# Two layers' product orders written out per 16 blocks, the negative part in three reduced-precision passes in every other block, and the last product with tokens on the partitions

## The chip, the cores and the metric

The kernel runs on one core of a Trainium2 chip (trn2). The metric is the device time of one execution in microseconds (us); the time of a kernel is the median over several executions. Inside a profile the time stands as a span, from the first to the last profiled instruction, which is about 2 us shorter than the device time of the same execution.

## The reference, cut to what matters

```python
# attention: 12288 queries, 768 pooled keys, width 128      -> x (12288 x 128)
h = x @ w_in1                                   # 128 -> 2048
x = (np.maximum(h, 0.0) + alpha * np.minimum(h, 0.0)) @ w_out1      # 2048 -> 128
h = x @ w_in2                                   # 128 -> 2048
P = a[0] + a[1] * h + a[2] * h**2 + a[3] * h**3
Q = 1.0 + np.abs(b[0]) * np.abs(h) + np.abs(b[1]) * h**2
return (P / (Q + 1e-06)) @ w_out2               # 2048 -> 128, float32
```

## The kernel before

All of x is kept in SBUF as two float32r halves, `x_hi` and `x_lo` (a rounded part and the rest), with the 128 features on the partitions. The attention fills it in the first fifth of the time. Then both layers run over 24 groups of 512 tokens; a group has 16 blocks of 128 hidden features, so each layer has 384 blocks. Every engine has its own instruction queue in one fixed order, and the queues meet through semaphores.

**Layer 1, block n.** TensorE: `hidden1(n)` (three float32r passes by `split_product`, L659 to L661) into the only PSUM bank `H1`. ScalarE takes its negative part `negative(n)` (L386); every fourth block VectorE does (L615). TensorE: `out1(n)` multiplies it by `wout1` in full float32 (L818) into `ACC1`, onto a linear term (`lin_hi`, `lin_lo`) that stands in for the rest of the activation. `hidden1(n+1)` waits until the negative part of block n is out of `H1`. After 16 blocks `hidden_hi` (ScalarE) and `hidden_lo` (VectorE) write the layer's output back to `x_hi`, `x_lo`.

**Layer 2, block m**, which runs `DEPTH` = 20 blocks behind. TensorE: `hidden2(m)` into one of three PSUM banks. ScalarE: `square` (L394), `scaled_abs` (L402), `linear_part` (L408). GpSimd: `cubic_term` (L256). VectorE: `denominator` (L577), `polynomial` (L583). ScalarE: `log` (L414), `inverse_q` (L422). VectorE: `check_product` (L600), `quotient` (L591). GpSimd: `correction` (L240), `final` (L248); in every fourth block VectorE does `final` (L608) and no correction is needed. TensorE: `out2(m)` (L829), full float32, into `ACC2`, with features on the partitions. `hidden2(m)` needs the quotient of block m-3, since there are three banks; `final(m)` needs `out2(m-3)`, since `rational` has three buffers.

**The output.** After 16 blocks ScalarE copies `ACC2` to `y_t` (`copy_output`), TensorE transposes it in four parts (`turn_output`, L835), VectorE copies it out (`place_output`, L627), and SyncE stores it.

A loop over periods of four blocks (`QUAD`) writes each engine's queue.

Of the kernel before, what the change touches and what calls it, by code (L numbers as in the profile page):

```python
# [13 lines left out]
P = 128  # L14
# [7 lines left out]
QUAD = 4  # L22
DEPTH = 5 * QUAD
BY_DVE_FINAL, BY_DVE_RELU = 2, 3
# [9 lines left out]
def build(nc, q, kv, w_sr, w_in1, w_out1, alpha, w_in2, w_out2, coef_p, coef_q, out):  # L34
# [7 lines left out]
    N1 = GROUPS * BLOCKS  # L42
# [11 lines left out]
    with ctx:  # L54
# [24 lines left out]
        with ExitStack() as scope:  # L79
# [4 lines left out]
            k_hi, k_lo = att("k_hi", [P, keys], F32R), att("k_lo", [P, keys], F32R)  # L84
            v_hi, v_lo = att("v_hi", [P, CHUNKS, P], F32R), att("v_lo", [P, CHUNKS, P], F32R)
            pt_hi, pt_lo = att("pt_hi", [P, 2, GROUP], F32R), att("pt_lo", [P, 2, GROUP], F32R)
            probs, expd = att("probs", [P, 2, TILES, keys]), att("expd", [P, 2, keys])
# [4 lines left out]
        y_t, y_out = sb("y_t", [P, GROUP]), sb("y_out", [P, GROUP])  # L92
# [24 lines left out]
        for name in (  # L117
# [5 lines left out]
            "in1_t_ready", "in1_t_done", "lin_ready", "lin_hi_done", "lin_lo_done", "out1_scaled",  # L123
# [4 lines left out]
            "h1_ready", "neg_done", "neg_dve_done", "m1_done", "y1_hi_done", "y1_done",  # L128
            "h2_ready", "sq_done", "absb_done", "linp_done", "cubic_done", "poly_done", "q_done", "ln_done", "rcp_done",
            "ratio_done", "qr_done", "newton_done", "rat_done", "rat_dve_done", "m2_done", "y2_copied", "y2_t_ready", "y2_out_done",  # L130
# [10 lines left out]
        def real(m):  # L141
            return 0 <= m < N1

        def group_at(p, offset):
            g = (p - offset) * QUAD // BLOCKS
            return g if (p - offset) * QUAD % BLOCKS == 0 and 0 <= g < GROUPS else None

        def negative_ready(eng, n):

            if n >= 0 and n % QUAD == BY_DVE_RELU:  # L150
                after(eng, s["neg_dve_done"], n // QUAD + 1)
            elif n >= 0:
                after(eng, s["neg_done"], n + 1 - (n + QUAD - BY_DVE_RELU) // QUAD)

        def rational_ready(eng, m):

            if m >= 0 and m % QUAD == BY_DVE_FINAL:
                after(eng, s["rat_dve_done"], m // QUAD + 1)
            elif m >= 0:
                after(eng, s["rat_done"], m + 1 - (m + QUAD - BY_DVE_FINAL) // QUAD)  # L160

        PERIODS = N1 // QUAD + DEPTH // QUAD + 2

# [27 lines left out]
        def _(pool):  # L191
# [45 lines left out]
            def correction(m):  # L237
                if real(m):
# [35 lines left out]
        def _(act):  # L274
# [160 lines left out]
            for p in range(PERIODS):  # L435
                n, m = p * QUAD, p * QUAD - DEPTH
                if group_at(p, 10) is not None:
                    copy_output(group_at(p, 10))
# [449 lines left out]
```

## Time and profile before

| | |
|---|---|
| median of 3 runs | 1619.42 us (1613.58 to 1620.19) |
| the profiled execution | 1616.42 us, span 1614.3 us |
| busy share of the span | TensorE 96%, VectorE 88%, ScalarE 87%, GpSimd 71% |

The shares are over the whole span with the attention in it, where GpSimd does little. In the trace an operation's record is longer than the step from its start to that of the next one, because operations are pipelined; the time that an operation takes from its engine is the step. In an entry such as `banks<-x_hi,win_lo` the output stands first. A full float32 matmul is two records, a float32r one is one record.

### The profile page before, as it was taken

How to read it: one execution, taken by the hardware profiler on the slowest of the kernel's cores; microseconds unless marked ns; L12 is line 12 of the kernel's file. 1: busy time of each engine (PE TensorE's matmuls, PEld its weight loads, DVE VectorE, ACT ScalarE, POOL GpSimd, SP SyncE). 2: the span in 40 equal slices, each digit the busy share in tenths (PEclk: the TensorE clock that was granted, in tenths of full speed). 3: DMA queues.
4: the chain of work that ended last, by engine and by line, in shares of the span. 5: the costliest groups of instructions: out<-in, count | busy, mean ns of one | idle time of the engine just before them, and what ended most of it. 6: DMA issues, size and time to landing. Idle time of an engine off the chain costs nothing. (4 is left out here: it accounts for less than half of the span.)

```text
span 1614.3 us, 22125 instructions
## 1 busy us (share of the span) xinstructions
PE 1555.7 (96%) x5869; PEld 1015.0 (63%) x5869; DVE 1412.7 (88%) x2175; ACT 1398.8 (87%) x2659; POOL 1149.2 (71%) x1256
## 2 busy tenths in 40 slices
PE   6899999989999999999999999999999999999976
PEld 5799999845566565655565555656656555656532
DVE  3688888727999999999999999999999999999997
ACT  2577777628999999999999999999999999999996
POOL 0344444306888888888888888888888888888887
PEclk9999999999999999999999999999999999999998
DMA  8110100000000000000000000000000000000000
GB/s 223 53 27 21 27 21 27 1 26 1 7 1 7 8 8 7 1 7 7 7 1 8 7 8 7 1 7 7 8 1 8 7 7 8 1 7 7 7 7 7
DMA packets 12299, 24.54 MB, mean 15 GB/s; under 512 B 1536, under 2 KB 1680, under 8 KB 11920
## 3 DMA queue, kind: packets, MB, share of 16 engines
q1 hardware_dynamic: 11424, 22.55, 4.7%
q8 instruction: 46, 0.75, 0.2%
q10 hardware_dynamic: 752, 0.60, 0.1%
q14 instruction: 77, 0.63, 0.1%
HBM read 16.85 MB, written 6.29 MB: 14 GB/s over the span
## 5 line engine op out<-in xcount | busy, mean ns | idle before, releaser
L256 POOL TENSOR_TENSOR cubic<-sq,lin_p 128x512 f32<-128x512 f32 x384 | 492.4, 1283 | 225.4 <-ACT lin_p L408 178.0
L659 PE MATMUL banks<-x_hi,win_lo 128*128 128x512 f32 x768 | 508.4, 662 | 25.2 <-DVE ratio L591 15.3
L248 POOL TENSOR_TENSOR rational<-newton,ratio 128x512 f32<-128x512 f32 x288 | 368.6, 1280 | 35.8 <-PE banks L829 13.6
L818 PE MATMUL banks<-neg_part,wout 128*128 128x512 f32 x768 | 388.0, 593 | 0.3 <-ACT neg_part L386 0.3
L829 PE MATMUL banks<-rational,wout 128*128 128x512 f32 x768 | 379.2, 601 | 4.2 <-POOL rational L248 4.1
L577 DVE SCALAR_TENSOR_TENSOR banks<-sq,abs_b,banks 128x512 f32<-128x512 f32 x384 | 282.3, 752 | 59.2 <-ACT banks L402 57.2
L661 PE MATMUL banks<-x_hi,win_hi 128*128 128x512 f32 x768 | 303.7, 395 | 0.0
L660 PE MATMUL banks<-x_lo,win_hi 128*128 128x512 f32 x768 | 303.3, 395 | 0.0
L591 DVE SCALAR_TENSOR_TENSOR ratio<-banks,ab_raw,rcp 128x512 f32<-128x512 f32 x384 | 285.5, 743 | 1.3 <-ACT rcp L422 1.2
L583 DVE SCALAR_TENSOR_TENSOR banks<-banks,ab_raw,cubic 128x512 f32<-128x512 f32 x384 | 280.0, 752 | 0.0
L659 PEld LDWEIGHTS banks<-x_hi,win_lo 128*128 128x128 f32 x768 | 145.1, 189 | 205.1 <-issue 67.7
L408 ACT ACTIVATE lin_p<-banks,ab_raw 128x512 f32<-128x512 f32 x384 | 267.2, 696 | 0.0
L394 ACT ACTIVATE sq<-banks 128x512 f32<-128x512 f32 x384 | 231.1, 602 | 37.6 <-PE banks L661 37.6
L422 ACT ACTIVATE rcp<-log_q 128x512 f32<-128x512 f32 x384 | 247.9, 646 | 3.1
L414 ACT ACTIVATE log_q<-banks 128x512 f32<-128x512 f32 x384 | 231.9, 604 | 2.3 <-DVE banks L577 2.2
L402 ACT ACTIVATE banks<-banks 128x512 f32<-128x512 f32 x384 | 223.4, 600 | 0.8 <-DVE newton L600 0.6
L660 PEld LDWEIGHTS banks<-x_lo,win_hi 128*128 128x128 f32 x768 | 145.8, 190 | 123.4 <-issue 115.9
L386 ACT ACTIVATE neg_part<-banks 128x512 f32<-128x512 f32 x288 | 175.2, 608 | 39.6 <-PE banks L661 29.3
L600 DVE SCALAR_TENSOR_TENSOR newton<-banks,rcp 128x512 f32<-128x512 f32 x288 | 197.3, 686 | 10.5 <-ACT rcp L422 7.5
L829 PEld LDWEIGHTS banks<-rational,wout 128*128 128x128 f32 x768 | 146.8, 192 | 90.2 <-issue 59.9
L818 PEld LDWEIGHTS banks<-neg_part,wout 128*128 128x128 f32 x768 | 142.6, 189 | 79.3 <-issue 54.1
L240 POOL TENSOR_SCALAR newton<-newton 128x512 f32<-128x512 f32 x288 | 178.0, 618 | 0.9 <-DVE newton L600 0.9
(84 smaller groups left out, 1891.1 us busy)
## 6 DMA issues: line engine op xcount, KB each, us to landing
early<-in_kv_dram SPq DMA_DIRECT2D x24, 256.0 KB, 9.6
out_dram<-y_out SPq DMA_DIRECT2D x24, 256.0 KB, 2.0
neg_part<-in_q_dram SPq DMA_DIRECT2D x22, 256.0 KB, 2.6
early<-in_moe_w_in_dram SPq DMA_DIRECT2D x1, 1024.0 KB, 5.5
wout<-in_moe_w_in_dram SPq DMA_DIRECT2D x1, 1024.0 KB, 4.8
neg_part<-in_q_dram ACTq DMA_DIRECT2D x2, 256.0 KB, 9.9
early<-in_w_sr_dram ACTq DMA_DIRECT2D x1, 64.0 KB, 5.7
wout<-in_moe_w_out_dram SPq DMA_DIRECT2D x2, 0.5 KB, 10.7
```

What stands on the lines that cost most here:

```text
L248: nc.gpsimd.tensor_tensor(rational[:, m % 3, :], newton[:, m % 2, :], ratio[:, m % 2, :], ALU.mult).then_inc(s["rat_done"], 1)
L256: nc.gpsimd.tensor_tensor(cubic[:, m % 2, :], sq[:, m % 2, :], lin_p[:, m % 2, :], ALU.mult).then_inc(s["cubic_done"], 1)
L408: nc.scalar.activation(lin_p[:, m % 2, :], banks[:, H2[m % 3], :], ACT.Identity, bias=ab_raw[:, 2:3], scale=scale_a3).then_inc(s["linp_don ...
L422: nc.scalar.activation(rcp[:, m % 2, :], log_q[:, m % 2, :], ACT.Exp, bias=float(-LN_SHIFT * np.log(2.0)), scale=-1.0).then_inc(s["rcp_don ...
L577: nc.vector.scalar_tensor_tensor(banks[:, QV[m % 2], :], sq[:, m % 2, :], abs_b[:, 1:2], banks[:, QV[m % 2], :], ALU.mult, ALU.add).then_i ...
L583: nc.vector.scalar_tensor_tensor(banks[:, H2[m % 3], :], banks[:, H2[m % 3], :], ab_raw[:, 1:2], cubic[:, m % 2, :], ALU.mult, ALU.add).th ...
L591: nc.vector.scalar_tensor_tensor(ratio[:, m % 2, :], banks[:, H2[m % 3], :], ab_raw[:, 0:1], rcp[:, m % 2, :], ALU.add, ALU.mult).then_inc ...
L659: nc.tensor.matmul(dst, w[1], x[0], start=start, stop=False)
L660: nc.tensor.matmul(dst, w[0], x[1], start=False, stop=False)
L661: return nc.tensor.matmul(dst, w[0], x[0], start=False, stop=stop)
L818: nc.tensor.matmul(banks[:, ACC1, :], wout1[:, c, :], neg_part[:, n % 2, :], start=False, stop=(c == BLOCKS - 1)).then_inc(s["m1_done"], 1)
L829: nc.tensor.matmul(banks[:, ACC2, :], wout2[:, c, :], rational[:, m % 3, :], start=(c == 0), stop=(c == BLOCKS - 1)).then_inc(s["m2_done"], 1)
```

## The change

- Layer 1, odd blocks (`SPLIT`): ScalarE writes the negative part as `neg_hi` in float32r, VectorE writes the rest as `neg_lo`, and `out1` is a `split_product` of three float32r passes with `wout1_hi`, `wout1_lo`. In even blocks it stays full float32. The first layer's input weights get their sign turned when they are split, so the negative part is a plain Relu. `neg_part`, `neg_hi` and `neg_lo` have two buffers each, for every other block.
- VectorE does the Relu in one block of 16 (`BY_DVE_RELU`, was four) and `final` in two (`BY_DVE_FINAL`, was four).
- `out2` has the `rational` tile as the stationary operand and 128 columns of `wout2` as the moving one, four matmuls a block; `ACC2` then has tokens on the partitions. `copy_output` and `turn_output` are gone, and `place_output` turns the sign.
- Each engine's queue is written out for a group of 16 blocks in place of four; layer 2 follows layer 1 by about 18 blocks.
- Before the layers ScalarE and VectorE also make `wout1_hi` and `wout1_lo` (1024 columns each).

```diff
-QUAD = 4
-DEPTH = 5 * QUAD
-BY_DVE_FINAL, BY_DVE_RELU = 2, 3
+BY_DVE_FINAL, BY_DVE_RELU = (4, 12), (14,)
+SPLIT = (1, 3, 5, 7, 9, 11, 13, 15)
...
+            act.wait_ge(s["out1_scaled"], 1)
+            act.wait_ge(s["s_ready"], GROUPS * TILES)
+            nc.scalar.activation(wout1_hi[:], wout1_odd, ACT.Copy).then_inc(s["out1_hi_done"], 1)
...
+                    after(act, s["m1_done"], n - 3)
+                    kept = neg_hi if c in SPLIT else neg_part
+                    nc.scalar.activation(kept[:, c // 2 % 2, :], banks[:, H1, :], ACT.Relu).then_inc(s["neg_done"], 1)
...
+            dve.wait_ge(s["out1_hi_done"], 1)
+            nc.vector.tensor_tensor(wout1_lo[:], wout1_odd, wout1_hi[:].bitcast(F32), ALU.subtract).then_inc(s["out1_lo_done"], 1)
...
+            def negative_lo(g, c):
+                if group(g):
+                    dve.wait_ge(s["neg_done"], made(g, c, BY_ACT_RELU))
+                    nc.vector.scalar_tensor_tensor(neg_lo[:, c // 2 % 2, :], banks[:, H1, :], 0.0,
+                                                   neg_hi[:, c // 2 % 2, :].bitcast(F32),
+                                                   ALU.max, ALU.subtract).then_inc(s["neg_lo_done"], 1)
...
+                    if c in SPLIT:
+                        split_product(banks[:, ACC1, :], (wout1_hi[:, h, :], wout1_lo[:, h, :]), (neg_hi[:, b, :], neg_lo[:, b, :]),
+                                      False, last).then_inc(s["m1_done"], 1)
+                    else:
+                        nc.tensor.matmul(banks[:, ACC1, :], wout1[:, c, :], neg_part[:, b, :], start=False,
+                                         stop=last).then_inc(s["m1_done"], 1)
...
-                    nc.tensor.matmul(banks[:, ACC2, :], wout2[:, c, :], rational[:, m % 3, :], start=(c == 0),
-                                     stop=(c == BLOCKS - 1)).then_inc(s["m2_done"], 1)
-
-            def turn_output(g):
-                pe.wait_ge(s["y2_copied"], g + 1)
-                for t in range(TILES):
-                    last = nc.tensor.transpose(banks[:, ACC2, t * P:(t + 1) * P], y_t[:, t * P:(t + 1) * P], ident[:])
-                last.then_inc(s["y2_t_ready"], 1)
...
+                    for t in range(TILES):
+                        last = nc.tensor.matmul(banks[:, ACC2, t * P:(t + 1) * P], rational[:, m % 3, t * P:(t + 1) * P], wout2[:, c, :],
+                                                start=(c == 0 and t == 0), stop=(c == BLOCKS - 1), skip_group_check=True)
+                    last.then_inc(s["m2_done"], 1)
```

TensorE's queue in the steady part of before, from one `hidden1` on. `win1`, `wout1` are layer 1's weights, `win2`, `wout2` layer 2's; the semaphore in brackets is what the row waits for.

```order
L659 MATMUL banks<-x_hi,win1_lo 128x512 [waits neg_done]
L660 MATMUL banks<-x_lo,win1_hi 128x512
L661 MATMUL banks<-x_hi,win1_hi 128x512
L818 MATMUL banks<-neg_part,wout1 128x512 [waits neg_done]
L659 MATMUL banks<-x_hi,win2_lo 128x512 [waits ratio_done]
L660 MATMUL banks<-x_lo,win2_hi 128x512
L661 MATMUL banks<-x_hi,win2_hi 128x512
L829 MATMUL banks<-rational,wout2 128x512 [waits rat_done]
L829 MATMUL banks<-rational,wout2 128x512 [waits rat_dve_done]
```

The same engine now, from the `out1` of block 5 to the `out2` of block 1:

```order
L846 MATMUL banks<-neg_hi,wout1_lo 128x512 [waits neg_lo_done]
L847 MATMUL banks<-neg_lo,wout1_hi 128x512
L848 MATMUL banks<-neg_hi,wout1_hi 128x512
L846 MATMUL banks<-x_hi,win1_lo 128x512 [waits neg_done]
L847 MATMUL banks<-x_lo,win1_hi 128x512
L848 MATMUL banks<-x_hi,win1_hi 128x512
L1025 MATMUL banks<-wout2,rational 128x128 [waits rat_done]
L1025 MATMUL banks<-wout2,rational 128x128 x3
L846 MATMUL banks<-x_hi,win2_lo 128x512 [waits ratio_done]
L847 MATMUL banks<-x_lo,win2_hi 128x512
L848 MATMUL banks<-x_hi,win2_hi 128x512
L1025 MATMUL banks<-wout2,rational 128x128 [waits rat_done]
```

One `out1` is three rows in place of one, and an `out2` is four matmuls of 128 columns in place of one of 512, with the operands changed over.

VectorE's queue before, from a `denominator` on, with its Relu and its `final`:

```order
L577 SCALAR_TENSOR_TENSOR banks<-sq,abs_b,banks 128x512 [waits sq_done,absb_done]
L615 TENSOR_SCALAR neg_part<-banks 128x512 [waits m1_done,h1_ready]
L591 SCALAR_TENSOR_TENSOR ratio<-banks,ab_raw,rcp 128x512 [waits rat_done,poly_done,rcp_done]
L600 SCALAR_TENSOR_TENSOR banks<-banks,rcp 128x512 [waits rcp_done]
L583 SCALAR_TENSOR_TENSOR banks<-banks,ab_raw,cubic 128x512 [waits cubic_done]
L608 SCALAR_TENSOR_TENSOR rational<-banks,ratio 128x512 [waits m2_done,ratio_done,qr_done]
```

And now, from `place_output`, which opens the group's order, to the second `negative_lo`:

```order
L760 TENSOR_SCALAR y_out<-banks 128x512 [waits st_out,m2_done]
L696 SCALAR_TENSOR_TENSOR banks<-sq,abs_b,banks 128x512 [waits sq_done,absb_done]
L704 SCALAR_TENSOR_TENSOR banks<-banks,ab_raw,cubic 128x512 [waits absb_done,cubic_done]
L745 SCALAR_TENSOR_TENSOR neg_lo<-banks,neg_hi 128x512 [waits neg_done]
L722 SCALAR_TENSOR_TENSOR newton<-banks,rcp 128x512 [waits rat_done,rcp_done]
L713 SCALAR_TENSOR_TENSOR ratio<-banks,ab_raw,rcp 128x512 [waits rat_done,poly_done,rcp_done]
L722 SCALAR_TENSOR_TENSOR newton<-banks,rcp 128x512 [waits rat_done,rcp_done]
L704 SCALAR_TENSOR_TENSOR banks<-banks,ab_raw,cubic 128x512 [waits absb_done,cubic_done]
L696 SCALAR_TENSOR_TENSOR banks<-sq,abs_b,banks 128x512 [waits sq_done,absb_done]
L713 SCALAR_TENSOR_TENSOR ratio<-banks,ab_raw,rcp 128x512 [waits rat_done,poly_done,rcp_done]
L696 SCALAR_TENSOR_TENSOR banks<-sq,abs_b,banks 128x512 [waits sq_done,absb_done]
L745 SCALAR_TENSOR_TENSOR neg_lo<-banks,neg_hi 128x512 [waits neg_done]
```

A `negative_lo` now stands in VectorE's queue once in every two blocks; it waits for ScalarE, and the next `hidden1` waits for it (`neg_lo_done`).

## Rows read from the trace of the kernel before

**Rows 1.** Busy time in stretches (PE, PEld, DVE, ACT, POOL), then granted clock, DMA.
```profile
420.00:1536.00 1116.00, 1112.60 (x3613) 667.17 (x3612) 1053.60 (x1601) 1068.62 (x2034) 926.60 (x865) 1.00 0.02 6
1555.00:1600.00 45.00, 32.15 (x78) 16.06 (x76) 42.48 (x65) 40.45 (x77) 39.04 (x38) 0.85 0.02 6
1600.00:1614.30 14.30, 7.28 (x12) 2.52 (x12) 6.11 (x10) 3.23 (x6) 5.89 (x6) 0.74 0.05 18
```

**Rows 2.** `place_output`, once a group: durations, first and last start.
```profile
L627 DVE COPY y_out<-banks x24: 681/684/692, 435.9 to 1611.0; 128x512 f32<-128x512 f32 x24
```

**Rows 3.** Waits from 900 to 1216 us: total us, times, longest.
```profile
POOL cubic L256 <- ACT lin_p L408: 32.4, 50, 1.3
...
PEld banks L659 <- DVE ratio L591: 7.6, 25, 0.5
```

**Rows 4.** Timeline of TensorE in the steady part: start, us, operation, count.
```profile
901.95 2.74 PE L829 MATMUL banks<-rational,wout 128*128 128x512 f32 x6
...
904.75 0.40 PE L660 MATMUL banks<-x_lo,win_hi 128*128 128x512 f32 x1
...
911.44 0.40 PE L659 MATMUL banks<-x_hi,win_lo 128*128 128x512 f32 x1
...
912.13 1.02 PE L818 MATMUL banks<-neg_part,wout 128*128 128x512 f32 x2
```

**Rows 5.** Float32 matmuls of 128 columns near the start: timeline, and durations (ns).
```profile
25.76 3.81 PE L711 MATMUL banks<-wout,early 128*128 128x128 f32 x32 [1.74 <-DMA wout<-in_moe_w_out_dram]
...
L711 PE MATMUL banks<-wout,early x32: 275/275/348, 25.8 to 29.3; 128*128 128x128 f32 x32
```

**Rows 6.** Timeline of VectorE in the steady part.
```profile
901.13 1.42 DVE L577 SCALAR_TENSOR_TENSOR banks<-sq,abs_b,banks 128x512 f32<-128x512 f32 x2
...
910.00 0.74 DVE L591 SCALAR_TENSOR_TENSOR ratio<-banks,ab_raw,rcp 128x512 f32<-128x512 f32 x1
910.66 0.69 DVE L600 SCALAR_TENSOR_TENSOR banks<-banks,rcp 128x512 f32<-128x512 f32 x1
911.26 0.75 DVE L583 SCALAR_TENSOR_TENSOR banks<-banks,ab_raw,cubic 128x512 f32<-128x512 f32 x1
911.91 0.68 DVE L608 SCALAR_TENSOR_TENSOR rational<-banks,ratio 128x512 f32<-128x512 f32 x1
912.51 0.68 DVE L600 SCALAR_TENSOR_TENSOR newton<-banks,rcp 128x512 f32<-128x512 f32 x1
```

**Rows 7.** Timeline of ScalarE: the first and the ninth of nine operations without a gap.
```profile
900.46 1.12 ACT L402 ACTIVATE banks<-banks 128x512 f32<-128x512 f32 x2
...
904.46 0.71 ACT L422 ACTIVATE rcp<-log_q 128x512 f32<-128x512 f32 x1
```

**Rows 8.** Timeline of GpSimd in the steady part.
```profile
919.00 0.62 POOL L240 TENSOR_SCALAR newton<-newton 128x512 f32<-128x512 f32 x1
919.70 1.27 POOL L248 TENSOR_TENSOR rational<-newton,ratio 128x512 f32<-128x512 f32 x1
920.93 1.29 POOL L256 TENSOR_TENSOR cubic<-sq,lin_p 128x512 f32<-128x512 f32 x1
```

**Rows 9.** Timeline of TensorE with layer 1 alone, and the first `hidden2` (last row).
```profile
340.29 0.49 PE L659 MATMUL banks<-x_hi,win_lo 128*128 128x512 f32 x1
...
341.93 0.50 PE L659 MATMUL banks<-x_hi,win_lo 128*128 128x512 f32 x1
...
369.47 0.40 PE L659 MATMUL banks<-x_hi,win_lo 128*128 128x512 f32 x1
```

**Rows 10.** Timelines of ScalarE and VectorE at the end of the attention.
```profile
329.70 1.90 ACT L311 ACTIVATE win_hi<-wout 128x2048 fp32r<-128x2048 f32 x1
...
321.35 2.28 DVE L569 TENSOR_TENSOR wout<-wout,one_minus_al 128x2048 f32<-128x2048 f32 x1
```

**Rows 11.** Timeline of the end: copy to `y_t`, and copy out.
```profile
1609.67 0.60 ACT L433 ACTIVATE y_t<-banks 128x512 f32<-128x512 f32 x1 [6.92 <-PE banks L829]
...
1611.03 0.69 DVE L627 COPY y_out<-banks 128x512 f32<-128x512 f32 x1 [5.47 <-PE banks L835]
```

More of the change, by code:

```diff
@@ L41, in build @@
     HALF = keys // 2
-    N1 = GROUPS * BLOCKS
     SCALE = float(1.0 / np.sqrt(d))
@@ L249, in final, with cubic_term @@
                                             ALU.mult).then_inc(s["rat_done"], 1)
-            def cubic_term(m):
-                if real(m):
+            def cubic_term(g, c):
+                if group(g):
+                    m = g * BLOCKS + c
                     pool.wait_ge(s["sq_done"], m + 1)
@@ L629, in _ @@
-            for p in range(PERIODS):
-                n, m = p * QUAD, p * QUAD - DEPTH
-                if group_at(p, 10) is not None:
-                    place_output(group_at(p, 10))
-                denominator(m)
-                if group_at(p, 4) is not None:
-                    hidden_lo(group_at(p, 4))
-                denominator(m + 1)
-                polynomial(m)
-                polynomial(m + 1)
-                quotient(m)
-                check_product(m)
-                check_product(m + 1)
-                quotient(m + 1)
-                denominator(m + 2)
-                polynomial(m + 2)
-                denominator(m + 3)
-                negative(n + 3)
-                quotient(m + 2)
-                check_product(m + 2)
-                polynomial(m + 3)
-                final(m + 2)
-                check_product(m + 3)
-                quotient(m + 3)
+                    after(dve, s["m1_done"], n - 3)
@@ new lines, in out2 @@
+                    last.then_inc(s["m2_done"], 1)
+            for p in range(GROUPS + 3):
+                hidden2(p - 3, 15)
+                hidden1(p - 1, 1)
+                out2(p - 3, 10)
+                out2(p - 3, 11)
+                hidden2(p - 2, 0)
+                out2(p - 3, 12)
+                linear(p - 1)
+                hidden1(p - 1, 2)
+                hidden2(p - 2, 1)
+                out1(p - 1, 0)
+                hidden1(p - 1, 3)
+                out2(p - 3, 13)
+                hidden2(p - 2, 2)
+                out1(p - 1, 1)
+                out2(p - 3, 14)
+                hidden1(p - 1, 4)
+                hidden2(p - 2, 3)
+                out2(p - 3, 15)
+                hidden1(p - 1, 5)
+                out1(p - 1, 2)
+                hidden2(p - 2, 4)
+                out1(p - 1, 3)
+                out1(p - 1, 4)
+                hidden1(p - 1, 6)
+                hidden2(p - 2, 5)
+                out1(p - 1, 5)
+                hidden1(p - 1, 7)
+                out2(p - 2, 0)
+                hidden2(p - 2, 6)
+                out2(p - 2, 1)
+                hidden1(p - 1, 8)
+                out1(p - 1, 6)
+                hidden2(p - 2, 7)
+                hidden1(p - 1, 9)
+                out2(p - 2, 2)
+                out1(p - 1, 7)
+                hidden2(p - 2, 8)
+                out2(p - 2, 3)
+                hidden1(p - 1, 10)
+                out2(p - 2, 4)
+                hidden2(p - 2, 9)
+                out1(p - 1, 8)
+                hidden1(p - 1, 11)
+                out1(p - 1, 9)
+                hidden2(p - 2, 10)
+                out2(p - 2, 5)
+                out1(p - 1, 10)
+                hidden1(p - 1, 12)
+                hidden2(p - 2, 11)
+                out2(p - 2, 6)
+                hidden1(p - 1, 13)
+                out2(p - 2, 7)
+                out1(p - 1, 11)
+                hidden2(p - 2, 12)
+                hidden1(p - 1, 14)
+                hidden2(p - 2, 13)
+                out2(p - 2, 8)
+                out1(p - 1, 12)
+                hidden1(p - 1, 15)
+                out1(p - 1, 13)
+                hidden2(p - 2, 14)
+                out1(p - 1, 14)
+                out2(p - 2, 9)
+                hidden1(p, 0)
+                out1(p - 1, 15)
```

504 lines of the change are left out of this document (337 added, 167 removed).

## The prediction

> **What bounds the kernel now.** I read four views. First the stretches: from 420 to 1536 us, where both layers run, TensorE is busy 1112.60 of 1116 us at full clock, VectorE 94%, ScalarE 96%, GpSimd 83% [rows 1]. A group of 16 blocks has 74 VectorE operations (four in each block, four `final`, four Relu, `hidden_lo`, `place_output`), and 1601 stand in the stretch: 21.64 groups, so **51.6 us a group**; `place_output` agrees with (1611.0 - 435.9) / 23 = 51.1, the faster drain included [rows 2]. Second the waits: GpSimd waits for ScalarE, 32.4 us in 316, while TensorE's wait for a quotient adds up to 7.6 us and is spent on weight loads [rows 3]. Third the timelines of the four engines, for the step of each operation. Fourth the start and the end, where the pipeline fills and drains.
>
> TensorE's steps [rows 4]: three float32r passes begin at 911.44 and the next matmul at 912.13, so 0.23 us a pass. Six float32 records and one pass lie between 901.95 and 904.75, so (2.80 - 0.23) / 6 = 0.43 a record, 0.86 a full product. A group has 96 passes of `hidden`, 32 full products, three passes of the linear term and four transposes (about 0.4 in all, an estimate): 22.2 + 27.4 + 0.7 + 0.4 = 50.7 us. Of the 51.6, 0.9 is waiting. TensorE is the bound, and a saving there counts until another engine is in the way.
>
> **TensorE after, per group.** (a) Eight `out1` go from 0.86 to three passes of 0.23: 8 x (0.86 - 0.69) = **-1.3 us**. (b) `out2`: four matmuls of 128 columns are eight records in place of two. Such products stand near the start, each with its own stationary tile: 32 records in 3.81 us, the last of which lasts 0.275, so (3.81 - 0.275) / 31 = 0.114 a record [rows 5]. Eight make 0.91 against 0.86, in 16 blocks **+0.9**. Its bounds: 0.107 (a quarter of 0.43, nothing lost to being short) gives 0, and 0.119 (3.81 / 32) gives +1.5. I take 0.114, the same form of instruction. (c) The transposes go: **-0.4**. Sum: **-0.8**, so 49.9 us, and 49.0 to 50.5 by the bounds.
>
> A rule speaks against (b). The weight load of a 128-column tile takes as long as the matmul here. The Trainium skill ("TensorE: Matmul & The Clock Gate", LDWEIGHTS) puts a load at the number of its columns divided by 1.2, about 107 ns, and its section on the back-to-back gap says that the spacing in a stream of load-and-matmul pairs is set by both. By the load alone the sum would be the same; with no overlap it would be 0.214 a record. The rows have 0.114 with a new tile for every product, so the load lies beside the matmul.
>
> **The other engines after, per group.** VectorE's steps: quotient 0.66, check 0.60, polynomial 0.65, final 0.60; the denominator's pair lasts 1.42, so 0.66 [rows 6]. Before: 16 x 2.57 + 8 x 0.60 + two of 0.65 = 47.2. The change takes two `final` and three Relu and adds eight `negative_lo`, which read one bank and one SBUF tile as `check_product` does: 0.60, with 0.66 as the upper bound. Net three more: **49.0 to 49.5**. ScalarE: nine starts span 4.00 us, so 0.50 an operation [rows 7]; 94 a group become 96 (three more Relu, `copy_output` gone): 47.0 to **48.0**. GpSimd: correction 0.70, final 1.23, cubic 1.26 [rows 8]; 16 cubics and 12 pairs make 43.3, with 14 pairs **47.2**.
>
> So four engines lie at 49.9, 49.3, 48.0 and 47.2. The busy ones have 0.6, 1.9 and 2.7 us to spare, where they had 4.4, 4.6 and 8.3. What the group takes is decided by whether the written-out order asks more than that of them in waits.
>
> **The order, laid out.** I put TensorE's rows of one group end to end with the steps above, time 0 at `hidden2` of the last block of the group before, and looked for the places with the least room. The bank `H1`: after a split block the way is 0.2 to ScalarE, 0.6, then VectorE 0.7 and 0.1 back, 1.6 us; between `hidden1(13)` and `hidden1(14)` stand an `out2`, an `out1` and a `hidden2`, 2.3 us, elsewhere 2.5 to 4. After an even block the way is 0.9 and 1.4 to 2.5 stand between. No wait there, if ScalarE and VectorE come to it in time. VectorE's order opens with `place_output`, which can begin when `out2(15)` ends, at 14.1; from there `quotient(2)` ends at 18.0 and `hidden2(5)`, which needs that bank, begins at 18.5; later quotients have 0.5 to 2 us. Three places cost: ScalarE is 0.5 late for VectorE around the first three blocks; `final(12)` on VectorE waits about 0.6 for `out2(9)` (three `rational` buffers), which stands near the end of TensorE's order; `final(13)` on GpSimd waits 1.8 for `out2(10)`, which stands in the next group's. Behind that one wait `cubic_term(15)` and then the first cubic; with 1.8 of 2.7 spent they still come before VectorE wants them. VectorE has spent 1.1 with 0.6 to spare: some half a microsecond is TensorE's. **49.9 + 0.6 = 50.5 us a group.** Before, the waits were 0.9; the same now would be 50.8.
>
> **The start.** `hidden1(0)` now waits for `wout1_lo`. ScalarE makes `wout1_hi` at 329.70, half of the 1.90 us that 2048 columns take, VectorE the rest in half of 2.28 [rows 10]: ready at 331.9. Block 1 begins about 333.4. With layer 1 alone a block takes 1.64 us [rows 9], and after a split one VectorE's 0.69 and 0.1 more, 2.4; 15 steps to block 16 make 8 x 2.4 + 7 x 1.64 = 30.7. Then `out1(15)`, `hidden_hi` and `hidden_lo` (3 us), and about 1 us for `out1` pairs in the way: the first `hidden2` at **368**, against 369.5 now [rows 9].
>
> **The end.** Layer 2 alone takes 45 us for 65 VectorE operations, 4.3 a block, so 3.0 us a block [rows 1]; GpSimd's 47.2 / 16 = 2.95 fits under it. Of 384 blocks 20 run alone now and 17 then. Before: 369.5 + 364 / 16 x 51.6 = 1543.4, 20 x 3.0 = 60, and 10.9 for the last chain. In the chain the copy to `y_t` and the transposes go, from 1609.67 to 1611.03, 1.4 us [rows 11]: 9.5. That TensorE's clock is down there (0.74, so partly at 1.2 GHz [rows 1]) holds for both kernels.
>
> **Sum.** 368.1 + 367 / 16 x 50.5 + 51 + 9.5 = 1587 us of span against 1614.3, 27 less. With 2.1 around it 1589 against 1616.4; the median of the runs lies 3.0 over the profiled execution, so **1593**. Each microsecond a group is worth 23.
>
> **Rivals.**
> 1. *The order holds all the way*, no waits: 49.9 a group, 1578. For it: the places above fit at that pace but for VectorE's half microsecond. Chance 0.12.
> 2. *Gain, but with waits as now or a little more*: 50.9 to 51.3, 1601 to 1611; part of the forecast's side. Against it stands only the layout.
> 3. *The gain is eaten*: waits of 1.4 to 2.1 us a group, 51.3 to 52.0, 1611 to 1627. Every hop that I took 0.1 too short comes up several times in a group. Chance 0.13.
> 4. *VectorE becomes the bound, slower.* `negative_lo` stands in VectorE's queue and waits for ScalarE; behind it wait check and quotient, for which TensorE waits. Eight stand in a group; if each holds VectorE 0.35 us beyond its room, the group takes 49.3 + 2.8 = 52.1 and the kernel 1629. It decides from 2.7 us a group. For it: VectorE has 0.6 to spare. Against: of eight places seven have ScalarE's Relu done when VectorE arrives, in the layout. Chance 0.15.
> 5. *Weight loads aren't hidden*: 16 x 8 x 0.1 = 12.8 us a group, 1886. Against it are the rows of 128 columns [rows 5]. The Trainium skill's rule on both operations setting the spacing would be this one at its worst. Chance 0.02.
>
> **Numbers.** The forecast with rival 2 holds 0.58 (50.3 to 51.3 a group, 1588 to 1611), rival 1 0.12. The range reaches from 1580 over the forecast and rival 3 to **1624**. A measurement tells from no change about 0.5%, 8 us: faster 0.70, within 0.13, slower 0.17.
>
> **What the profile would show.** `place_output` every 50.5 us (51.6 now). Records of `out2`: eight a block at 0.114. `out1` of odd blocks in 0.7. VectorE at 97 to 98%, GpSimd at 93%, TensorE as full as now. The first `hidden2` by 368, and no ScalarE or TensorE record between the last `out2` and `place_output`. Wrong if: the step of `out2` is over 0.125 (rival 5 in part); `hidden1` or `hidden2` begin late behind `neg_lo` or `ratio` by over 1.5 us a group; or VectorE's own steps grow with GpSimd fuller.

## The result, and the profile after

The median is 1571.22 us (1570.87 to 1571.82, four runs) against 1618.54 us for the kernel before (1613.58 to 1620.19): a ratio of **0.9713, with an interval from 0.9691 to 0.9735**, 2.9% faster. The forecast was 1593, with a range from 1580 to 1624: the sign was right, the size lies 9 us below the range. The profiled execution took 1570.87 us, its span 1568.7.

First the busy time of the stretch in which both layers run (same columns as [rows 1]), then `place_output`, which answers to [rows 2]:

```profile
385.00:1500.00 1115.00, 1115.00 (x6000) 904.39 (x5999) 1110.15 (x1730) 1109.76 (x2158) 1039.80 (x990) 1.00 0.02 6
```

```profile
L760 DVE TENSOR_SCALAR y_out<-banks x24: 677/681/691, 429.0 to 1565.4; 128x512 f32<-128x512 f32 x24
```

TensorE's records cover all 1115.00 of 1115 us. That alone doesn't show that it never waits: its records last about 0.40 us where the steps are 0.23, so a short wait hides under the overlap. The kernel below with one more ScalarE operation behind `scaled_abs(3)` has the same work on TensorE and a group 0.49 us longer, and the same stretch of it reads just as full:

```profile
385.00:1500.00 1115.00, 1115.00 (x5942) 891.92 (x5941) 1104.75 (x1713) 1109.79 (x2159) 1029.00 (x979) 1.00 0.02 6
```

Whether anything waits is read from the time of a group against the sum of the steps. For the time of a group I take `hidden_lo`, which writes `x_lo` once a group; 22 of them start between 400 and 1500 us, 21 groups apart. Before, and then after:

```profile
L621 DVE TENSOR_TENSOR x_lo<-banks,x_hi x22: 684/685/686, 410.9 to 1495.0; 128x512 fp32r<-128x512 f32 x22
```

```profile
L753 DVE TENSOR_TENSOR x_lo<-banks,x_hi x22: 682/684/685, 416.9 to 1459.8; 128x512 fp32r<-128x512 f32 x22
```

Before (1495.0 - 410.9) / 21 = 51.62 us, after (1459.8 - 416.9) / 21 = **49.66 us a group**. Of 384 blocks 367 run so, 22.9 groups: 1.96 x 22.9 = 45 of the 45.6 us by which the span is shorter. Counted with 22.9 groups in both, start and end together take 430 us in both.

TensorE in the steady part, which answers to [rows 4]:

```profile
900.66 1.05 PE L1025 MATMUL banks<-wout,rational 128*128 128x128 f32 x8
901.47 0.49 PE L846 MATMUL banks<-neg_hi,wout_lo 128*128 128x512 f32 x1
901.79 0.40 PE L847 MATMUL banks<-neg_lo,wout_hi 128*128 128x512 f32 x1
...
902.27 0.39 PE L846 MATMUL banks<-x_hi,win_lo 128*128 128x512 f32 x1
...
902.96 0.39 PE L846 MATMUL banks<-x_hi,win_lo 128*128 128x512 f32 x1
```

Three float32r passes take 902.96 - 902.27 = 0.69, so 0.23 each. From 900.66 to 901.79 lie eight records of `out2` and one pass: (1.13 - 0.23) / 8 = 0.1125 a record. A group's work is then 123 passes of 0.23 (28.3), 16 records of 0.43 for the eight full `out1` (6.9) and 128 of 0.1125 (14.4): 49.6, which is the measured group to 0.1. This sum is what shows that TensorE waits for next to nothing.

VectorE at `final(12)` and GpSimd at `final(13)`, the two places where the prediction saw waits:

```profile
909.50 0.74 DVE L713 SCALAR_TENSOR_TENSOR ratio<-banks,ab_raw,rcp 128x512 f32<-128x512 f32 x1
910.33 0.69 DVE L731 SCALAR_TENSOR_TENSOR rational<-banks,ratio 128x512 f32<-128x512 f32 x1
```

```profile
913.92 1.29 POOL L254 TENSOR_TENSOR rational<-newton,ratio 128x512 f32<-128x512 f32 x1 [0.93 <-PE banks L1025]
```

A quotient takes 0.66, so `final(12)` starts 0.17 late, not 0.6; GpSimd waits 0.93, not 1.8. The `out2(9)` that the prediction had `final(12)` wait for is already done, at 909.01 + 1.05 = 910.06:

```profile
909.01 1.05 PE L1025 MATMUL banks<-wout,rational 128*128 128x128 f32 x8
```

The waits from 700 to 1100 us, eight groups (columns as in [rows 3]):

```profile
POOL rational L254 <- PE banks L1025: 7.7, 8, 1.1
...
PEld banks L846 <- ACT neg_part L431: 4.4, 16, 0.4
...
PEld banks L846 <- DVE neg_lo L745: 3.4, 8, 0.5
PEld banks L846 <- DVE ratio L713: 2.3, 10, 0.3
```

TensorE's are on weight loads (PEld) alone, at most 0.5 us, and by the sum above the matmuls in front cover them. GpSimd's 32.4 us of waiting for `linear_part` [rows 3] are gone, and VectorE has no row in this view. The start, TensorE's rows of the first blocks and the first `hidden2`:

```profile
330.95 0.48 PE L846 MATMUL banks<-x_hi,win_lo 128*128 128x512 f32 x1 [3.09 <-DVE wout_lo L688]
...
332.59 0.80 PE L846 MATMUL banks<-x_hi,win_lo 128*128 128x512 f32 x1 [0.69 <-ACT neg_part L431]
333.18 0.63 PE L847 MATMUL banks<-x_lo,win_hi 128*128 128x512 f32 x1
...
338.96 0.40 PE L847 MATMUL banks<-x_lo,win_hi 128*128 128x512 f32 x1
...
369.13 0.50 PE L846 MATMUL banks<-x_hi,win_lo 128*128 128x512 f32 x1 [0.46 <-DVE x_lo L753]
```

TensorE stands still for 3.09 us until `wout1_lo` is there, and from 332.6 on its records last 0.63 where they last 0.40 elsewhere. The clock granted in that stretch is 0.50 (column behind the five engines):

```profile
332.50:338.50 6.00, 5.78 (x12) 3.61 (x12) 1.83 (x2) 1.23 (x3) 0.00 (x0) 0.50 0.51 159
339.00:345.00 6.00, 4.59 (x18) 2.81 (x16) 1.38 (x2) 1.79 (x3) 0.00 (x0) 1.00 0.00 0
```

### The profile page after: what moved, and what is told of

Read it like the earlier page. It is cut to its first block and busy times, and to the rows that moved or that the text cites. A ratio compares the mean times of both kernels' runs of the same rounds, so it can differ in the third digit from the quotient of the medians.

```text
span 1568.7 us, 28339 instructions
## 1 busy us (share of the span) xinstructions
PE 1517.8 (97%) x8269; PEld 1250.2 (80%) x8269; DVE 1434.0 (91%) x2248; ACT 1401.9 (89%) x2708; POOL 1232.9 (79%) x1352
## 5 line engine op out<-in xcount | busy, mean ns | idle before, releaser
L254 POOL TENSOR_TENSOR rational<-newton,ratio 128x512 f32<-128x512 f32 x336 | 434.0, 1292 | 29.4 <-PE banks L1025 21.1
L1025 PEld LDWEIGHTS banks<-wout,rational 128*128 128x128 f32 x3072 | 402.6, 193 | 43.4 <-issue 11.0
L846 PE MATMUL banks<-x_hi,win_lo 128*128 128x512 f32 x768 | 387.9, 505 | 23.6 <-DVE ratio L713 11.6
L1025 PE MATMUL banks<-wout,rational 128*128 128x128 f32 x3072 | 405.3, 277 | 3.0 <-POOL rational L254 3.0
L449 ACT ACTIVATE banks<-banks 128x512 f32<-128x512 f32 x384 | 267.8, 697 | 2.9 <-DVE rational L731 1.8
L464 ACT ACTIVATE log_q<-banks 128x512 f32<-128x512 f32 x384 | 263.5, 686 | 4.8 <-DVE banks L696 4.6
L439 ACT ACTIVATE sq<-banks 128x512 f32<-128x512 f32 x384 | 266.3, 694 | 0.8 <-PE banks L848 0.7
L245 POOL TENSOR_SCALAR newton<-newton 128x512 f32<-128x512 f32 x336 | 209.4, 623 | 22.0 <-DVE newton L722 12.6
L1015 PE MATMUL banks<-neg_part,wout 128*128 128x512 f32 x384 | 196.8, 594 | 0.0
L848 PEld LDWEIGHTS banks<-x_hi,win_hi 128*128 128x128 f32 x768 | 144.8, 188 | 32.9
L745 DVE SCALAR_TENSOR_TENSOR neg_lo<-banks,neg_hi 128x512 fp32r<-128x512 f32 x192 | 130.9, 682 | 25.5 <-ACT neg_hi L431 25.4
```

The source lines that it names most:

```text
L254: nc.gpsimd.tensor_tensor(rational[:, m % 3, :], newton[:, m % 2, :], ratio[:, m % 2, :], ALU.mult).then_inc(s["rat_done"], 1)
L449: nc.scalar.activation(banks[:, QV[m % 2], :], banks[:, H2[m % 3], :], ACT.Abs, scale=scale_b0).then_inc(s["absb_done"], 1)
L846: nc.tensor.matmul(dst, w[1], x[0], start=start, stop=False)
L848: return nc.tensor.matmul(dst, w[0], x[0], start=False, stop=stop)
L1025: last = nc.tensor.matmul(banks[:, ACC2, t * P:(t + 1) * P], rational[:, m % 3, t * P:(t + 1) * P], wout2[:, c, :], start=(c == 0 and t == ...
```

## The experiments

Each is an edit of the changed kernel, of the kernel before in two cases. Single runs are compared by the time of a group, from `hidden_lo` as above; a single span carries some microseconds of the start and the end besides (the first `hidden_lo` after 400 us starts between 413.6 and 421.5 in the single runs on the changed kernel).

**Which part brings what.** Four kernels: the new order alone (1), with the token-major output but no split (2), with the split but the old output (3), and the old order with only the new output (4).

```diff
-SPLIT = (1, 3, 5, 7, 9, 11, 13, 15)                      # 1, 2: all out1 in full float32,
+SPLIT = ()                                               # no negative_lo on VectorE
...
+                copy_output(p - 3)                       # 1, 3: on ScalarE behind scaled_abs(3),
+                turn_output(p - 3)                       # on TensorE behind out1(2),
-                place_output(p - 3)                      # on VectorE
+                place_output(p - 3)                      # behind quotient(2)
...
-                    nc.tensor.matmul(banks[:, ACC2, :], wout2[:, c, :], rational[:, m % 3, :], ...)
+                    for t in range(TILES):               # 4: before, with the four small matmuls
+                        last = nc.tensor.matmul(banks[:, ACC2, t * P:(t + 1) * P], rational[:, m % 3, t * P:(t + 1) * P], ...)
```

> The written-out order alone: no split (the odd blocks' negative part stays full float32, in a tile of its own), output product with features on the partitions and its copy and transposes put into the order. Theory A, that the order itself took the 1.1 us a group that TensorE waited before: 50.5 us a group (TensorE's work: 99 passes at 0.2305, 64 records at 0.4265, transposes 0.35), span 1584. Theory B, that the waits went because TensorE had less to do and other engines were rebalanced: 51.4 to 51.6 a group, span 1605 to 1610.

> The changed kernel without the split, so that only the order and the token-major output product are there. Theory A: TensorE's work is 22.8 + 13.65 + 14.4 = 50.9 us a group and nothing waits, span about 1592, 23 above the changed kernel. Theory B: 51.5 or more a group, span 1606 and up.

> The changed kernel with the output product as before (features on the partitions, copy and transposes in the order): what the token-major form is worth. By TensorE's work it costs 14.4 - 13.65 - 0.35 = 0.4 us a group, so without it 49.2 a group and a span near 1561, 0.5% faster than the changed kernel. Rival: VectorE (49.0 of work) and the longer output chain eat that, 49.6 a group and a span of 1570.

> The kernel before with the token-major output product alone. Theory A: +0.75 - 0.35 us a group on TensorE, waits as before: 51.95 to 52.0 a group, 1.4 less at the end, span about 1621. Rival: the copy and transposes were behind the waits, and with them gone the group takes 51.3 or less, span 1607 or less.

`hidden_lo` of the first three:

```profile
L753 DVE TENSOR_TENSOR x_lo<-banks,x_hi x22: 682/684/685, 416.5 to 1483.8; 128x512 fp32r<-128x512 f32 x22
```

```profile
L746 DVE TENSOR_TENSOR x_lo<-banks,x_hi x22: 684/684/684, 416.3 to 1485.5; 128x512 fp32r<-128x512 f32 x22
```

```profile
L760 DVE TENSOR_TENSOR x_lo<-banks,x_hi x22: 681/684/686, 418.1 to 1472.6; 128x512 fp32r<-128x512 f32 x22
```

| kernel | span | us a group |
|---|---|---|
| before | 1614.3 | 51.62 |
| 4: old order, new output | 1611.3 | 51.58 |
| 1: new order alone | 1594.7 | 50.82 |
| 2: new order and output, no split | 1595.2 | 50.91 |
| 3: new order and split, old output | 1582.8 | 50.21 |
| after: all three | 1568.7 | 49.66 |

Kernel 1 has the products of the kernel before, and by the steps above they are 99 passes of 0.23, 64 records of 0.43 and some 0.4 of transposes, 50.7: its group takes its TensorE work, to 0.1 (kernel 2 too: 22.8 + 13.8 + 14.4 = 51.0). So the kernel before waited 51.62 - 50.82 = 0.8 us a group, and the order alone (with its moved Relus and `final`s, which no run separates from it) takes all of that away.

The split brings 1.25 where the output is the new one, of the 1.3 or so that it saves on TensorE. The new output brings nothing without the split: kernel 2 differs from kernel 1 by it alone and takes 0.09 more, which is what it adds to TensorE's work. With the split it brings 0.55.

Of my four expectations only kernel 2's figure for a group (50.9) came out. Kernel 1 lies between its two theories, kernel 4 between its two; kernel 3 was to take 49.2 or 49.6. Its TensorE work is 49.66 - 0.09 = 49.6, so it waits about 0.6; its waits from 700 to 1100 us:

```profile
PEld banks L853 <- DVE ratio L720: 15.9, 40, 0.6
...
PEld banks L853 <- DVE neg_lo L752: 12.3, 24, 0.9
...
PEld banks L853 <- ACT neg_part L431: 9.5, 39, 0.3
```

Against 2.3, 3.4 and 4.4 after: with copy and turn in the queues every hand-over comes a little late. Over four runs kernel 3 takes 1587.20 us (1581.91 to 1589.84), 0.9807 of before (0.9779 to 0.9834). So on top of the split the token-major output is worth 14 us of span, by what it takes from ScalarE and from the chain, while it costs TensorE 0.09 us a group.

Whether 0.6 is the price of copy and turn or of where I put them, the next one asks: the copy one operation earlier, `place_output` behind `quotient(3)`.

> The feature-major variant of the changed kernel again, with ScalarE's copy one operation earlier and VectorE's place_output behind the quotient of block 3 instead of block 2. If the loss of 14 us in that variant is one of placing these operations, this one moves towards TensorE's work, 49.3 a group, span 1562 to 1575. If the loss is due to the operations themselves, it stays at 1580 to 1585.

Span 1602.8, 51.08 a group (1072.6 / 21): worse by 0.9. It is outside both of my ranges. TensorE's weight loads now wait 8.3 us in 400 for `place_output`. The places of two operations are worth as much as the whole wait of the kernel before, so the 14 us hold for my placement.

**The split in the old order.** Kernel 4 with the split in odd blocks, two `negative_lo` in each period of four; VectorE's Relu goes to ScalarE.

```diff
                 denominator(m + 3)
-                negative(n + 3)
+                negative_lo(n + 3)
...
                 polynomial(m + 1)
+                negative_lo(n + 1)
                 quotient(m)
```

> The kernel before with both new forms of product (split in odd blocks, token-major output) in its old order of four blocks: ScalarE takes all Relus, VectorE eight negative_lo and four final a group. TensorE's work is the changed kernel's, 49.6. If the new forms are what counts, it takes 50 a group or less, span 1580. If the order is needed to use them (one H1 bank, now held by two engines in a row, in an order laid out for one), the waits of 1 us before grow: 51 to 52.5 a group, span 1600 to 1635.

Span 1786.0, 58.9 us a group, far outside what either theory gave. Waits from 700 to 1100 us:

```profile
POOL cubic L260 <- ACT lin_p L415: 75.5, 55, 1.9
PEld banks L664 <- DVE ratio L595: 31.7, 55, 0.8
PEld banks L664 <- DVE neg_lo L618: 31.6, 34, 1.6
```

All engines idle in turn. It is one placement of several possible ones, so it doesn't show that the split needs the new order; it shows that the split without a fitting order can cost 170 us.

**What room is left.** Four kernels add work to the changed one, once a group: one VectorE operation behind `quotient(8)`, ahead of `negative_lo(11)`; one ScalarE operation behind `scaled_abs(3)`; three passes on TensorE (the linear term twice; the second product starts the sum anew, so the output is the same); and the ScalarE operation ahead of `log(12)` instead. The added engine operations write a tile that nobody reads.

```diff
+                    nc.vector.scalar_tensor_tensor(scratch[:], win2_hi[:, 0:GROUP].bitcast(F32), 1.0, win2_lo[:, 0:GROUP].bitcast(F32),
+                                                   ALU.mult, ALU.add)
...
+                    nc.scalar.activation(scratch[:], win2_hi[:, 0:GROUP].bitcast(F32), ACT.Copy)
...
+                    split_product(banks[:, ACC1, :], (lin_hi[:], lin_lo[:]), (x_hi[:, cols], x_lo[:, cols]), True, True)
```

> The changed kernel with one more VectorE operation a group (0.60 us, SBUF only, into a tile that nobody reads), behind the quotient of block 8: how much room VectorE has. As the prediction laid it out (0.6 us of room, 1.1 us of waits, which add up) it is full and the group grows by the whole 0.6, span 1568.7 + 14 = 1583. If waits of different places don't add up (a lateness from one place covers the next), there is 49.57 - 49.0 = 0.57 of room: 0 to 0.2 a group, span 1569 to 1573.

> The changed kernel with one more ScalarE operation a group (0.5 us, SBUF only, no waits), where the copy of the output stood in the feature-major variant, behind the scaled_abs of block 3. If the copy on ScalarE is what cost the feature-major variant its 0.9 us a group of waits: span 1583 or more. If ScalarE has its 1.3 us of room (49.57 - 48.3): span 1569 to 1571.

> The changed kernel with the linear term of layer 1 computed twice, so three more float32r passes on TensorE a group (0.69 us): is TensorE alone the bound. If it is, the group takes 50.26 and the span is 1584.6. If VectorE, ScalarE or a ring through all of them sets the pace beside it, part of the 0.69 is covered: span under 1580.

> The extra ScalarE operation of 0.5 us a group again, now ahead of the log of block 12, where ScalarE waits 0.3 to 0.4 us for VectorE. If ScalarE is full as a whole: 0.5 a group, span 1580, as at the first place. If the room at the place counts: 0.1 to 0.2 a group, span 1570 to 1574.

| added | span | us a group | growth |
|---|---|---|---|
| VectorE 0.67, behind `quotient(8)` | 1582.3 | 50.24 | 0.58 |
| ScalarE 0.5, behind `scaled_abs(3)` | 1580.5 | 50.15 | 0.49 |
| TensorE 0.69 | 1584.6 | 50.29 | 0.63 |
| ScalarE 0.5, ahead of `log(12)` | 1569.4 | 49.66 | 0.00 |

TensorE is the bound, so the group grows by nearly all of its addition. But it grows by nearly all of VectorE's too and, at one place, of ScalarE's: the three go in lockstep. That an operation of ScalarE is free ahead of `log(12)` and costs its whole length behind `scaled_abs(3)` shows that a sum of idle time over a group is no measure of room; the place is. With VectorE's addition TensorE waits where that operation stood ahead, from 700 to 1100 us:

```profile
PEld banks L852 <- DVE neg_lo L745: 8.6, 8, 1.1
```

**One more VectorE operation, at `final(12)`.** There the trace showed VectorE 0.17 early, so it should have been the cheap place.

> The extra VectorE operation of 0.60 us a group again, now ahead of the final of block 12, where VectorE waits 0.1 to 0.2 us for TensorE anyway. If VectorE is full as a whole, the group grows by 0.6 wherever the operation stands: span 1582. If only the room at the place counts (the wait of 0.17, and 0.3 between hidden_lo and the hidden2 that needs it), it grows by 0.15 to 0.4: span 1572 to 1578.

Span 1596.0, 50.80 a group: 1.14 more, twice the growth at the other place and against my expectation. VectorE's and GpSimd's timelines there:

```profile
922.87 1.41 DVE L758 SCALAR_TENSOR_TENSOR scratch<-win_hi,win_lo 128x512 f32<-128x512 f32 x1
924.21 0.68 DVE L731 SCALAR_TENSOR_TENSOR rational<-banks,ratio 128x512 f32<-128x512 f32 x1
```

```profile
922.45 1.29 POOL L254 TENSOR_TENSOR rational<-newton,ratio 128x512 f32<-128x512 f32 x1
923.70 1.74 POOL L263 TENSOR_TENSOR cubic<-sq,lin_p 128x512 f32<-128x512 f32 x1
```

The added operation takes 1.34 instead of 0.67 and ends 0.5 us after GpSimd's instruction, which had begun before it; GpSimd's next one lasts 1.74 in place of 1.29. Either the place or the two SBUF operands could be why. Two kernels tell: the same place with one SBUF source, and with a PSUM bank and an SBUF tile, as all of the kernel's own have (`final(12)` computed once more into an unread tile).

```diff
+                    nc.vector.tensor_scalar(scratch[:], win2_hi[:, 0:GROUP].bitcast(F32), 1.0, None, ALU.mult)
...
+                    nc.vector.scalar_tensor_tensor(scratch[:], banks[:, QV[m % 2], :], 2.0, ratio[:, m % 2, :],
+                                                   ALU.subtract, ALU.mult)
```

> The changed kernel plus an extra VectorE operation ahead of final(12), where the same place with two SBUF sources cost 1.2 us a group (span 1596) and lasted up to 1.43 us. Here it reads one SBUF source. If reading two SBUF operands beside GpSimd is what stretched it, its duration is near 0.6 to 0.75 and the growth at most 0.6 a group: span at most 1582. If the place alone costs that much, or if any read of SBUF beside GpSimd is stretched, it is again near 1596.

> The changed kernel plus an extra VectorE operation ahead of final(12), at the place where operations on SBUF alone cost 1.2 us a group (two sources, step 1.34) and 0.6 a group (one source, step 1.08). Here it reads a PSUM bank and one SBUF tile, as all of the kernel's own do: it computes final(12) once more into a tile that nobody reads. If those two were held up by GpSimd's instruction on SBUF and the place itself is like any other, the step is 0.60 at every place, GpSimd's next cubic stays at 1.28, and the growth is at most 0.6 less the 0.17 that VectorE waits there: span 1579 to 1583. If the place is what costs, it is near 1596 again.

The timeline of the one-source kernel, VectorE and then GpSimd:

```profile
914.15 1.16 DVE L758 TENSOR_SCALAR scratch<-win_hi 128x512 f32<-128x512 f32 x1
915.23 0.68 DVE L731 SCALAR_TENSOR_TENSOR rational<-banks,ratio 128x512 f32<-128x512 f32 x1
```

```profile
913.72 1.31 POOL L254 TENSOR_TENSOR rational<-newton,ratio 128x512 f32<-128x512 f32 x1
914.97 1.50 POOL L263 TENSOR_TENSOR cubic<-sq,lin_p 128x512 f32<-128x512 f32 x1
```

And VectorE's with the bank, from the quotient on:

```profile
918.83 0.74 DVE L713 SCALAR_TENSOR_TENSOR ratio<-banks,ab_raw,rcp 128x512 f32<-128x512 f32 x1
919.67 0.69 DVE L761 SCALAR_TENSOR_TENSOR scratch<-banks,ratio 128x512 f32<-128x512 f32 x1
920.28 0.68 DVE L731 SCALAR_TENSOR_TENSOR rational<-banks,ratio 128x512 f32<-128x512 f32 x1
```

| source of the added operation | its step | us a group | growth | added to VectorE's queue there |
|---|---|---|---|---|
| two SBUF tiles | 1.34 | 50.80 | 1.14 | 1.17 |
| one SBUF tile | 1.08 | 50.49 | 0.83 | 0.91 |
| a bank and an SBUF tile | 0.61 | 50.19 | 0.53 | 0.61 |

The last column is the step, less the 0.17 of idle time where the operation fills it. The one with the bank doesn't: it reads the quotient's result itself and starts 919.67 - 918.83 = 0.84 behind it, 0.18 late, and `final` then follows without a gap. The growth follows that column to 0.1. With a bank the operation has its ordinary 0.61, and the growth falls to that of the other place: it was the operands, not the place.

My expectation for one source was wrong, it is held up as well: its shortest record in the kernel is 0.57 us, the median 1.16. The expectation for the bank kernel gives one source 0.6 a group, by the spans; by `hidden_lo` it is 0.83. The bank kernel's span is 1586.0, over the 1579 to 1583 expected, with a start that took some 5 us longer (first `hidden_lo` at 421.5 against 416.9).

The Trainium skill ("SBUF — State Buffer", Who interferes with whom) has both: a VectorE instruction with two SBUF inputs, beside a GpSimd one that reads SBUF, or a single-source one that uses both of VectorE's ports, contends with GpSimd for a port pair that they share, and whichever begins first holds it. The timelines agree: in both the added operation ends 0.3 to 0.5 us behind the end of GpSimd's earlier instruction, not within it.

**The gap ahead of `final`.** The prediction put it down to `out2` three blocks back. Four `rational` buffers in place of three, with the addition behind `quotient(8)`:

```diff
-                    after(dve, s["m2_done"], m - 2)
-                    nc.vector.scalar_tensor_tensor(rational[:, m % 3, :], ...
+                    after(dve, s["m2_done"], m - 3)
+                    nc.vector.scalar_tensor_tensor(rational[:, m % 4, :], ...
```

> The changed kernel plus an extra VectorE operation after quotient(8), as in the earlier run that cost 13.6 us, and rational with four buffers in place of three. If the waits of VectorE's two final operations (0.17 and 0.12 us in the trace, for an out2 three blocks back) are what uses up its room, taking them away gives back up to 0.3 us a group: 49.57 + 0.3 = 49.9, span about 1575. If those waits only stand for being early, and the ring through TensorE, VectorE and ScalarE has no room whatever the buffer, the extra operation costs the full 0.6 again: span about 1582.

Span 1580.7, 50.25 a group, as with three buffers, and the gap is the same to the hundredth:

```profile
914.92 0.74 DVE L713 SCALAR_TENSOR_TENSOR ratio<-banks,ab_raw,rcp 128x512 f32<-128x512 f32 x1
915.75 0.69 DVE L731 SCALAR_TENSOR_TENSOR rational<-banks,ratio 128x512 f32<-128x512 f32 x1
```

So it isn't the buffer. `final(12)` stands right behind the quotient whose result it reads. The last two kernels move both `final`s behind the next polynomial, without and with the addition:

```diff
                 quotient(p - 2, 12)
-                final(p - 2, 12)
                 polynomial(p - 2, 13)
+                final(p - 2, 12)
```

> The changed kernel with VectorE's two final operations one place later, behind the next polynomial, so that neither stands right behind the operation whose result it reads. If the gaps of 0.17 and 0.12 us ahead of them are the wait for that result, which four rational buffers left as they were, final starts 0.66 us after the polynomial with no gap. TensorE has no gap to give back, so the group stays at 49.66 us and the span within 3 us of 1568.7. If the later rational or the earlier polynomial holds up a neighbour, a group grows by up to 0.3: 1575.

> The same, with the extra VectorE operation after quotient(8) that cost 0.58 us a group (1055.1 us for 21 groups). If VectorE's idle time in a group is one sum, the 0.29 us freed at the two final operations pays for half of it: 49.95 us a group, 1049 us for 21 groups, span about 1576. If room counts only at its place, the extra operation costs 0.58 again: 50.24 a group, span about 1582.

```profile
917.17 0.75 DVE L704 SCALAR_TENSOR_TENSOR banks<-banks,ab_raw,cubic 128x512 f32<-128x512 f32 x1
917.83 0.68 DVE L731 SCALAR_TENSOR_TENSOR rational<-banks,ratio 128x512 f32<-128x512 f32 x1
```

The gap is gone, so it was a wait of VectorE for its own last result. But the group takes 50.20 us, 0.54 more than with the gap, and 50.80 with the addition; both are over what I expected. Waits of the first from 700 to 1100 us:

```profile
PEld banks L846 <- ACT neg_part L431: 10.7, 24, 0.6
...
PEld banks L846 <- DVE neg_lo L745: 7.2, 16, 0.7
PEld banks L846 <- DVE ratio L713: 6.6, 21, 0.4
...
ACT banks L449 <- DVE rational L731: 2.1, 8, 0.3
```

ScalarE now waits for `final` (last row), and TensorE's weight loads wait 10.7 us for the Relu where they waited 4.4. ScalarE's 0.26 a group is only half of the 0.54, so the waits don't show the whole chain. An idle 0.29 us on VectorE was taken out, and the kernel became 12.7 us slower.

**A better start.** `wout1_hi`, `wout1_lo` and the splitting of `win2` move behind the first Relus, and TensorE waits for `wout1_lo` only at `out1(1)`.

```diff
-            for name in ("in1_lo_done", "lin_lo_done", "out1_scaled", "out1_lo_done"):
+            for name in ("in1_lo_done", "lin_lo_done", "out1_scaled"):
...
+                    if g == 0 and c == 1:
+                        pe.wait_ge(s["out1_lo_done"], 1)
```

> A version that should beat both: the changed kernel with wout1_hi, wout1_lo and the split of the second layer's input weights moved behind the first Relus, so that the first hidden1 need not wait for them. The first hidden1 begins where the attention ends, 3.2 us earlier (327.7 for 330.95), and TensorE is not idle long enough there to fall to half its clock, which stood in the changed kernel's rows from 333 to 338 and cost 2 us: span 1563.5, 0.3% faster. If the split of the weights then holds up the first blocks instead: 1566 to 1570.

```profile
326.99 0.39 PE L850 MATMUL banks<-x_hi,win_lo 128*128 128x512 f32 x1
...
328.68 0.49 PE L850 MATMUL banks<-x_hi,win_lo 128*128 128x512 f32 x1 [0.83 <-ACT neg_part L427]
...
363.19 0.50 PE L850 MATMUL banks<-x_hi,win_lo 128*128 128x512 f32 x1 [0.46 <-DVE x_lo L752]
```

`hidden1(0)` stands right behind the attention's last matmul, no record is stretched, and the first `hidden2` comes at 363.2 instead of 369.1, as expected. Over four runs: **1566.01 us** (1563.98 to 1568.66), 0.9681 of before (0.965 to 0.9711). Its span of 1561.8 is 6.9 us under after's, the median 5.2; the group stays at 49.66. It is the best version of all.

## Why the prediction missed

- **The bound: right.** TensorE was it, and the group now takes its work to 0.1.
- **TensorE's work: 0.3 us too much, mostly in the output.** The split gives what was said: 1.25 against 1.3. The output form was put at +0.9 for `out2` and -0.4 for the transposes, 0.5 in all; kernels 1 and 2, which differ by it alone, are 0.09 apart. `out2` has 0.1125 a record, where the rows near the start gave 0.114, and the rest is in steps read to 0.01 and multiplied by up to 128. Against that the old work was put 0.1 too low, 50.7 where kernel 1 takes 50.82. 49.6 in place of 49.9 is 6.6 us of the span.
- **The waits: the step that failed.** "VectorE has spent 1.1 with 0.6 to spare: some half a microsecond is TensorE's" made 50.5; TensorE waits for next to nothing. 0.55 x 22.9 = 12.6 us, the largest part of the miss. The 1.1 was 0.6 of `final(12)` for `out2(9)` and 0.5 of ScalarE's lateness, and neither came. `out2(9)` is done 0.27 us before `final(12)` starts, and the 0.17 by which that is late is the wait for its own quotient, which a fourth buffer leaves as it is. For ScalarE, VectorE has no row among the waits from 700 to 1100 us (before it had 19.0 us of them for `scaled_abs` alone). Why the layout, made with every engine on time, had both isn't settled; my reading is that it added waits at different places of one ring, where a delay at one uses up the next, and no run tests that by itself. That VectorE has next to no room was right: an operation of 0.67 more costs 0.58.
- **GpSimd's wait at `final(13)`: right in kind**, 0.93 for 1.8, and it stays within its own room.
- **The start: right to 1 us, by luck.** 369.1 against 368.1, with the attention's end 1.3 us earlier than in the profile before. The stretch of TensorE's slower clock from 332.6 to 338.9 wasn't in the sum.
- **The end: right.** 369.1 + 22.94 x 49.66 = 1508.3, and 60.4 to the end of the span, where 51 + 9.5 was forecast.
- **The median over the profiled execution: wrong.** 3.0 us were carried over from before; it is 0.35. The four runs of after lie within 1 us, those of before within 7.
- **The rivals.** Rival 1, no waits, is what happened; its 1578 less the 6.6 us of work is about what was measured. It had 0.12, because one layout of the queues, with VectorE's half microsecond in it, outweighed the rest. Rival 4 (VectorE the bound, slower) is nearer than its time of 1629 looks: one VectorE operation of 0.67 more a group, or both `final`s one place later, gives back over a quarter of the gain.

The chain by which the split fits in the new order and not in the old one isn't settled beyond the waits shown, since only one placement was run.

## What to carry to other kernels

A layout of fixed queues tells where an engine may wait, but don't add up the waits of different places: here 1.1 us of them were laid out for VectorE, with 0.6 to spare, and TensorE lost next to nothing. Laying it out over several groups with the delays carried on, until it repeats, should do better; that wasn't tried here. Don't judge room by an engine's idle sum either: here 0.5 us of ScalarE was free at one place and cost all at another, and filling a 0.29 us gap cost 12.7 us. A busy share of 100% doesn't rule out waits either; compare the time of a group with the sum of its steps. And take the split, the order and the output form together: the order alone brought 0.8 us a group, the output alone nothing, the split on top of the order 0.6, all three 1.96, and the split in the old order, in the one placement that was run, cost 170 us in all.

## What the runs showed of the hardware

- A VectorE operation of 128 x 512 float32 with both operands in SBUF took 0.75 us or 1.43, one with a single SBUF source 0.57 or 1.16, the longer one where a GpSimd tensor operation had begun 0.4 us before it. Behind `quotient(8)`, 0.15 us ahead of GpSimd's next one and with GpSimd's one before at its last 0.2 us, the two-source operation kept 0.75, and GpSimd's next lasted 1.73 in place of 1.29. One that reads a PSUM bank and an SBUF tile kept 0.69 in all 24 cases.
- A VectorE operation that reads what the one right ahead of it has written begins 0.12 to 0.17 us late (`final(4)` and `final(12)`); with a polynomial in between, `final(12)` had no gap.
- After 3.09 us without work and one block's `hidden1`, TensorE was granted a clock of 0.50 for 6 us, the lower of its two levels (1.2 of 2.4 GHz). Without that pause, as in the last experiment, the clock was 1.00 from 327 to 345 us.
- A float32r pass of 512 columns takes 0.23 us here in a stream without gaps (three in 0.69). The Trainium skill ("TensorE: Matmul & The Clock Gate", Back-to-back issue gap) has about 0.131 for a matmul of that width in a sustained stream; no row here comes near that, and the measurement decides.
